# RWKV-style scan and two feed-forward blocks on one core: own terms and the one-token level of a tile from one product instead of two

## The chip, the cores and the metric

One NeuronCore of a Trainium2 chip runs the whole program. The metric is the device time of one execution in microseconds. Three runs of the kernel before gave 417.12, 417.32 and 419.42 us, so the time before is 417.32 us (median). All arithmetic is fp32 or a split of fp32 into two parts for TensorE.

## The reference

Inputs are r, k, v, w of shape (2 batches, 8 heads, 768 tokens, 48 features) and u of (8, 48).

```python
for t in range(S):
    cur = np.einsum('bhd,bhe->bhde', u[None] * kt, vt)
    y[:, :, t] = np.einsum('bhd,bhde->bhe', rt, state + cur)
    state = wt[:, :, :, None] * state + np.einsum('bhd,bhe->bhde', kt, vt)
```

So y at token t is a sum over earlier tokens s of (r_t, decayed k_s) v_s, where the decay is the product of w over the tokens strictly between s and t, and an **own term** (r_t, u k_t) v_t. For s = t - 1 no decay stands between them. After this come a normalised feed-forward block on 384 features (width 1536, relu, added to its input), and a second block with a product over the 768 tokens; neither is touched by the change.

## The kernel before

The 2 x 768 tokens are cut into 12 tiles of 128 tokens (NT = 12). In a tile the scores between tokens are built in levels c = 1, 2, 4, ... 64 (LEVELS): level c pairs the left half of every run of 2c tokens (keys) with its right half (queries). Between two levels DVE multiplies the right halves of r by the decay of a run (r_right, lines 824, 826, 821) and POOL the left halves of k (k_left, lines 559, 561, 556), in place, so the next level starts only when both are done, and both start only when TensorE (PE) has read the level before.

On PE a level (near_level, line 1120) is 16 matmuls: 4 pairs of heads, two blocks of 64 tokens, two halves of the array. Each loads 64 columns of k and streams the 32 odd columns of r in the block. The product lands in PSUM (tiles low_bank, odd_bank, high_bank), and DVE copies the entries that belong to the level into the tile near with a masked copy (select, line 868). The last level is far_level (line 1134), which ScalarE (ACT) copies to the tile score (place_blocks, line 668).

The own term has a pass of its own: ACT makes uk = u times k (own_k, line 623, four activations of 128 elements), PE multiplies uk by r in 16 matmuls of 64 columns (own_term, line 1082), and DVE copies the diagonal out with a mask over all 64 columns (own_select, line 838, 512 elements a partition). ACT then copies near to score (place_near, line 654), widens the state (widen, line 678), and PE forms y of the tile from wide and score (attend, lines 1164 and 1168) and turns k (turn_k, line 1147). A state update (gain, line 1177) and a transposition of the normalised x (turn, line 1195) follow in later slots.

The order is written out by hand for each engine: all walk through 52 slots k = 4s + j (slots_of_scan). In slot (s, j) PE does low level j of tile s, then one high level of tile s - 1; at j = 3 also the own term of tile s + 1, the attend and turn_k of tile s - 1. ACT makes uk for tile s + 1 at j = 1 and place_blocks, place_near and widen at j = 2. From slot 20 on (s = 5) each slot also holds one step of the first feed-forward block (first_product and second_product, lines 1201 to 1203) on PE; this stretch is called **beside** below, and slots 0 to 19 (tiles 0 to 4, ALONE = 4) **alone**. Weights are split in two parts by ACT (weight_hi, line 644) and POOL (weight_lo, line 571) in between. Every engine runs its own list in order.

Of the kernel before, what the change touches and what calls it, by code (L numbers as in the profile page):

```python
# [29 lines left out]
P = 128  # L30
# [3 lines left out]
Q = 64  # L34
# [9 lines left out]
def rwkv_moe_kernel(nc, rT, kT, wT, v, u, g_ln, w1, w2, w_in, w_sp, b_sp, w_out, masks, ident, out):  # L44
# [18 lines left out]
    with ExitStack() as ctx:  # L63
# [42 lines left out]
        uk = place("uk", [P, NPR, P])  # L106
# [42 lines left out]
        def low_pair(i, n):  # L149

            return (odd if i <= ALONE and n % 2 else low)[:, :, 0:Q // 2]

        def own_pair(i):

            return (high if i <= ALONE + 1 else low)[:, :, Q:2 * Q]
# [80 lines left out]
        uk_ready = sem("uk_ready")  # L236

        own_done = sem("own_done")
        low_done = sem("low_done")
        high_done = sem("high_done")  # L240
        own_placed = sem("own_placed")
# [295 lines left out]
        def _(pool):  # L537
            gp = nc.gpsimd

            def k_left(i, n):  # L540
# [8 lines left out]
                if i == n == 0:  # L549
                    pool.wait_ge(uk_ready, 1)  # L550
# [61 lines left out]
        def _(act):  # L612
            sc = nc.scalar

            def own_k(i):

                k_loaded(act, i)
                if i == 0:
                    act.wait_ge(u_loaded, 16)
                else:  # L620
                    act.wait_ge(own_done, i)
                for a in range(NPR):
                    last = sc.activation(uk[:, a, :], kin[i % 4][:, a, :], ACT.Identity, scale=ucol[:, a:a + 1])  # L623
                last.then_inc(uk_ready, 1)
# [23 lines left out]
            def place_near(i):  # L648
# [3 lines left out]
                act.wait_ge(own_placed, i + 1)  # L652
# [51 lines left out]
            own_k(0)  # L704
            for k, s, j in slots_of_scan():
# [4 lines left out]
                if j == 1 and s + 1 < NT:  # L710
                    own_k(s + 1)
# [63 lines left out]
        def _(dve):  # L775
# [29 lines left out]
            def r_right(i, n):  # L805
# [8 lines left out]
                if i == n == 0:  # L814
                    dve.wait_ge(own_done, 1)
# [13 lines left out]
            def own_select(i):  # L829

                if i == 0:
                    dve.wait_ge(near_zeroed, 2)
                    dve.wait_ge(consts_loaded, 48)
                if i >= 2:
                    dve.wait_ge(near_placed, i - 1)
                dve.wait_ge(own_done, i + 1)
                mk = msk[:, N_MASKED * Q // 2:]
                ve.copy_predicated(near[i % 2][:, :, :], mk[:, None, :].to_broadcast([P, H, Q]),
                                   own_pair(i)).then_inc(own_placed, 1)

            def select(i, n):

                c = LEVELS[n]
                if n == 0:
                    dve.wait_ge(own_placed, i + 1)
# [7 lines left out]
                if n == N_LOW - 1 and ALONE < i < NT - 1:  # L853
                    dve.wait_ge(own_done, i + 2)
# [4 lines left out]
                if c == 1:  # L859
                    dst = dst[:, :, :, 0]  # L860
                    mb = mk[:, None, :].to_broadcast([P, H, m])
                elif m == 1:
# [103 lines left out]
            for k, s, j in slots_of_scan():  # L966
# [4 lines left out]
                if k == 0:  # L971
                    own_select(0)
                if s < NT:
                    select(s, j)
                if j == 3 and s + 1 < NT:
                    own_select(s + 1)
# [94 lines left out]
        def _(te):  # L1071
            def own_term(i):

                k_loaded(te, i)
                r_loaded(te, i)
                te.wait_ge(uk_ready, i + 1)
                if 2 <= i <= ALONE + 1:
                    te.wait_ge(blocks_placed, i - 1)
                for a in range(NPR):
                    for s0 in range(0, P, Q):  # L1080
                        for e, (lo, hi) in enumerate(HALF):
                            mm = te.matmul(own_pair(i)[s0:s0 + Q, NPR * e + a, :], uk[lo:hi, a, s0:s0 + Q],
                                           rin[i % 4][lo:hi, a, s0:s0 + Q], start=True, stop=True)
                mm.then_inc(own_done, 1)

            def near_level(i, n):

                c = LEVELS[n]
                if n:
                    r_ready(te, i, n - 1)  # L1090
                    k_ready(te, i, n - 1)
                else:
                    k_loaded(te, i)
                    r_loaded(te, i)
# [3 lines left out]
                elif n < N_LOW:  # L1098
                    te.wait_ge(low_placed, N_LOW * i + n)
                    if n == 0 and i > ALONE + 1:  # L1100
# [286 lines left out]
```

## Time and profile before

| what | us |
|---|---|
| median of three runs | 417.32 |
| the profiled execution | 417.79 |
| its span, first to last instruction | 416.0 |
| PE busy | 391.5 |
| DVE, ACT, POOL busy | 226.8, 147.4, 127.4 |

The profiled execution took 417.79 us by the clock of the device, 1.8 us more than the span of its instructions. PE is the engine with the highest share, but the share is not even: the first 70 us hold most of its gaps. PE and PEld are the matmuls and the weight loads of the same engine, which overlap. Every matmul on fp32 data is counted twice (two passes), so a group of 16 shows as x32.

### The profile page before, as it was taken

The numbers are of one execution on the slowest core, as the hardware profiler recorded it, in microseconds if no ns is written. First come the engines' busy times: TensorE is split into PE (matmuls) and PEld (weight loads), VectorE is DVE, ScalarE is ACT, GpSimd is POOL, SyncE is SP. The second block draws the span as 40 slices with busy tenths as digits, with TensorE's granted clock in tenths as the row PEclk, the third lists the DMA queues.
The fourth block names the chain that finished last, engine by engine and source line by source line (L and its number), as shares of the span: only waits on it lengthen the run. The fifth ranks groups of instructions, "written<-read, shape, count | busy, mean of one in ns | idle before, by whom it ended". The sixth has DMA issues, their size and how long they took to land.

```text
span 416.0 us, 12346 instructions
## 1 busy us (share of the span) xinstructions
PE 391.5 (94%) x5244; PEld 371.0 (89%) x5244; DVE 226.8 (55%) x503; ACT 147.4 (35%) x328; POOL 127.4 (31%) x149
## 2 busy tenths in 40 slices
PE   3677788999999999999999999999999999999997
PEld 2666677999999999999999998998999899999996
DVE  2868778757576766666743334134126876624240
ACT  3334454362533333333234342222225743222121
POOL 4657667736362323232312241001003530000000
PEclk9997875999999999999999999999999999999999
DMA  6924532504201111020000210000033200010102
GB/s 199 325 63 136 172 83 96 173 2 136 73 28 45 30 47 27 4 96 4 2 2 2 70 48 0 0 2 0 2 104 125 76 2 0 2 57 3 57 19 96
DMA packets 26695, 24.99 MB, mean 60 GB/s; under 512 B 1680, under 2 KB 23440, under 8 KB 26640
## 3 DMA queue, kind: packets, MB, share of 16 engines
q1 hardware_dynamic: 26640, 24.19, 18.9%
q8 instruction: 42, 0.69, 0.7%
q14 instruction: 13, 0.11, 0.1%
HBM read 21.83 MB, written 2.36 MB: 58 GB/s over the span
## 4 chain that ended last, share of the span: by engine, by line
PE 91%; issue 3%; DVE 2%; POOL 2%; DMA 1%; ACT 0%; SPq 0%; DVEq 0%; POOLq 0%; ACTq 0%
PE odd_bank L1201 11%; PE odd_bank L1203 9%; PE odd_bank L1202 9%; PE low_bank L1120 7%; PE low_bank L1203 6%; PE low_bank L1201 6%; PE low_bank L1202 6%; PE high_bank L1201 4%; PE high_bank L1202 4%; PE high_bank L1203 4%; PE bank L1168 3%; PE bank L1203 3%; PE bank L1201 3%; PE bank L1202 3%; PE bank L1164 3%
## 5 line engine op out<-in xcount | busy, mean ns | idle before, releaser
L561 POOL TENSOR_TENSOR kin<-kin,wtot 128x256 f32<-128x256 f32 x60 | 48.5, 814 | 66.9 <-PE low_bank L1120 62.4
L1120 PEld LDWEIGHTS low_bank<-rin,kin 64*64 64x64 f32 x1728 | 31.8, 143 | 19.7 <-issue 8.1
L1120 PE MATMUL low_bank<-rin,kin 64*64 64x32 f32 x1728 | 36.3, 228 | 13.3 <-DVE rin L826 5.7
L826 DVE TENSOR_TENSOR rin<-rin,wtot 128x256 f32<-128x256 f32 x60 | 36.5, 612 | 15.5 <-PE low_bank L1120 13.4
L940 DVE SCALAR_TENSOR_TENSOR h10l<-odd_bank,h10h 128x384 fp32r<-128x384 f32 x24 | 13.4, 558 | 41.7 <-ACT h10h L700 41.7
L578 POOL TENSOR_TENSOR vrstd<-vmv,half 128x1 f32<-128x1 f32 x12 | 7.7, 644 | 72.0 <-DVE vmv L1023 72.0
L559 POOL TENSOR_TENSOR kin<-kin,win 128x256 f32<-128x256 f32 x12 | 13.1, 1089 | 49.5 <-PE low_bank L1120 45.9
L868 DVE COPY_PREDICATED near<-msk,low_bank 128x256 f32<-128x256 int32 x54 | 27.0, 552 | 0.0
L700 ACT ACTIVATE h11h<-odd_bank 128x384 fp32r<-128x384 f32 x16 | 7.9, 492 | 47.7 <-PE odd_bank L1203 47.7
L1201 PE MATMUL odd_bank<-xnT0h,ffw 128*128 128x384 f32 x66 | 24.4, 369 | 0.0
L1202 PE MATMUL odd_bank<-xnT0l,ffw 128*128 128x384 f32 x66 | 22.1, 336 | 0.0
L1203 PE MATMUL odd_bank<-xnT0h,ffw 128*128 128x384 f32 x66 | 22.1, 335 | 0.0
L1168 PE MATMUL bank<-vin,score 128*64 128x48 f32 x384 | 21.1, 245 | 0.0
L700 ACT ACTIVATE h10h<-odd_bank 128x384 fp32r<-128x384 f32 x24 | 11.8, 491 | 25.5 <-PE odd_bank L1203 25.3
L1201 PE MATMUL odd_bank<-xnT1h,ffw 128*128 128x384 f32 x54 | 19.7, 366 | 0.0
L1168 PEld LDWEIGHTS bank<-vin,score 128*64 128x64 f32 x384 | 19.5, 165 | 0.2
L1202 PE MATMUL odd_bank<-xnT1l,ffw 128*128 128x384 f32 x54 | 18.1, 336 | 0.0
L1203 PE MATMUL odd_bank<-xnT1h,ffw 128*128 128x384 f32 x54 | 18.1, 336 | 0.0
L623 ACT ACTIVATE uk<-kin,ucol 128x128 f32<-128x128 f32 x48 | 15.3, 392 | 5.7 <-DMA kin<-in_kT 2.9
L571 POOL TENSOR_TENSOR ffw<-early_stage,ffw 128x384 fp32r<-128x384 f32 x16 | 16.9, 1058 | 0.0
L1164 PE MATMUL bank<-wide,rin 128*64 128x96 f32 x160 | 16.8, 293 | 0.0
L1201 PE MATMUL high_bank<-ffw,h10h 128*128 128x384 f32 x48 | 16.1, 336 | 0.1
(244 smaller groups left out, 1138.3 us busy)
## 6 DMA issues: line engine op xcount, KB each, us to landing
kin<-in_kT SPq DMA_DIRECT2D x12, 256.0 KB, 3.3
rin<-in_rT SPq DMA_DIRECT2D x12, 256.0 KB, 4.7
win<-in_wT SPq DMA_DIRECT2D x12, 256.0 KB, 5.1
early_stage<-in_w SPq DMA_DIRECT2D x8, 384.0 KB, 5.1
vin<-in_v SPq DMA_DIRECT2D x12, 192.0 KB, 3.7
out<-ob SPq DMA_DIRECT2D x12, 192.0 KB, 1.9
stage<-in_w SPq DMA_DIRECT2D x4, 384.0 KB, 5.4
stage<-in_w_in SPq DMA_DIRECT2D x4, 384.0 KB, 3.4
```

Of the source, the lines that this page charges most:

```text
L561: last = gp.tensor_tensor(k, k, wr[:, :, :, None].to_broadcast([P, NPR, m, c]), ALU.mult)
L571: op = gp.tensor_tensor(lo[:, cs], slots[slot_of[n]][:, cs], hi[:, cs].bitcast(F32), ALU.subtract)
L623: last = sc.activation(uk[:, a, :], kin[i % 4][:, a, :], ACT.Identity, scale=ucol[:, a:a + 1])
L700: sc.activation(h1[n % 2][0][:, :], f1_bank(n)[:, 0:GT], ACT.Relu).then_inc(h1_hi_ready, 1)
L826: last = ve.tensor_tensor(r, r, wl[:, :, :, None].to_broadcast([P, NPR, m, c]), ALU.mult)
L868: ve.copy_predicated(dst, mb, src).then_inc(low_placed if n < N_LOW else middle_placed, 1)
L1120: mm = te.matmul(dst[s0:s0 + Q, NPR * e + a, :], kin[i % 4][lo:hi, a, s0:s0 + Q], r[:, :, 1, :], start=True, stop=True)
L1164: te.matmul(b_y[lo:hi, at:at + 2 * HD], rin[i % 4][:, a, lo:hi], wide[:, a, :], start=True, stop=False)
L1168: mm = te.matmul(b_y[lo:hi, at + e * HD:at + (e + 1) * HD], score[:, NPR * e + a, lo:hi], vin[i % 3][:, 2 * a + e, :], start=first(i), sto ...
L1201: te.matmul(o, wh, xh, start=first, stop=False)
L1202: te.matmul(o, wh, xl, start=False, stop=False)
L1203: return te.matmul(o, wl, xh, start=False, stop=last)
```

## The change

The own term and level c = 1 become one product. ACT writes two new tiles: k_first, which is k at even tokens and u times k at odd ones, and r_first, which is u times r at even tokens and r at odd ones. PE multiplies them in 16 matmuls of 64 columns into low_bank (first_level). At odd t the product with s = t is (r_t, u k_t) and with s = t - 1 it is (r_t, k_s); at even t the one with s = t is (u r_t, k_t). DVE takes those entries with one masked copy of 512 elements, and the mask of line 1342 gets the entries s + 1 = t at odd t. own_term, own_select and the semaphores own_done, own_placed and uk_ready go.

```diff
-            def own_k(i):
+            def first_terms(i):
                 k_loaded(act, i)
                 if i == 0:
                     act.wait_ge(u_loaded, 16)
                 else:
-                    act.wait_ge(own_done, i)
+                    act.wait_ge(low_done, N_LOW * (i - 1) + 1)
+                src, dst = halves(kin[i % 4][:, :, :], 1), halves(k_first[:, :, :], 1)
+                sc.copy(dst[0][:, :, :, 0], src[0][:, :, :, 0])
                 for a in range(NPR):
-                    last = sc.activation(uk[:, a, :], kin[i % 4][:, a, :], ACT.Identity, scale=ucol[:, a:a + 1])
-                last.then_inc(uk_ready, 1)
+                    sc.activation(dst[1][:, a, :, 0], src[1][:, a, :, 0], ACT.Identity, scale=ucol[:, a:a + 1])
+                r_loaded(act, i)
+                src, dst = halves(rin[i % 4][:, :, :], 1), halves(r_first[:, :, :], 1)
+                sc.copy(dst[1][:, :, :, 0], src[1][:, :, :, 0])
+                for a in range(NPR):
+                    last = sc.activation(dst[0][:, a, :, 0], src[0][:, a, :, 0], ACT.Identity, scale=ucol[:, a:a + 1])
+                last.then_inc(first_ready, 1)
...
-            def own_term(i):
-                k_loaded(te, i)
-                r_loaded(te, i)
-                te.wait_ge(uk_ready, i + 1)
-                if 2 <= i <= ALONE + 1:
-                    te.wait_ge(blocks_placed, i - 1)
+            def first_level(i):
+                te.wait_ge(first_ready, i + 1)
+                if i:
+                    te.wait_ge(low_placed, N_LOW * i - (1 if i <= ALONE else 0))
...
-                            mm = te.matmul(own_pair(i)[s0:s0 + Q, NPR * e + a, :], uk[lo:hi, a, s0:s0 + Q],
-                                           rin[i % 4][lo:hi, a, s0:s0 + Q], start=True, stop=True)
-                mm.then_inc(own_done, 1)
+                            mm = te.matmul(low_pair(i, 0)[s0:s0 + Q, NPR * e + a, :], k_first[lo:hi, a, s0:s0 + Q],
+                                           r_first[lo:hi, a, s0:s0 + Q], start=True, stop=True)
+                mm.then_inc(low_done, 1)
...
-                if s < NT:
+                if s < NT and j == 0:
+                    first_level(s)
+                elif s < NT:
                     near_level(s, j)
-                    if k == 0:
-                        own_term(0)
-                    if j == 3 and s + 1 < NT:
-                        own_term(s + 1)
```

On DVE, own_select (line 838) and its two calls go, and select of level 0 takes the 512 elements with the wider mask. The waits on own_done, own_placed and uk_ready in k_left, r_right, select, place_near, near_level and second_product go with them.

PE at the program's start, tile 0 and the beginning of tile 1, before (kin_53 and rin_49 are k and r of tile 0, kin_54 and rin_50 of tile 1):

```order
1 L1120 MATMUL low_bank<-rin_49,kin_53 64x32 x16
2 L1082 MATMUL high_bank<-rin_49,uk 64x64 x16
3 L1120 MATMUL odd_bank<-rin_49,kin_53 64x32 x16
4 L1120 MATMUL low_bank<-rin_49,kin_53 64x32 x16
5 L1120 MATMUL odd_bank<-rin_49,kin_53 64x32 x16
6 L1082 MATMUL high_bank<-rin_50,uk 64x64 x16
7 L1120 MATMUL low_bank<-rin_50,kin_54 64x32 x16
8 L1120 MATMUL high_bank<-rin_49,kin_53 64x32 x16
```

and in the changed kernel:

```order
1 L1067 MATMUL low_bank<-r_first,k_first 64x64 x16
2 L1097 MATMUL odd_bank<-rin_49,kin_53 64x32 x16
3 L1097 MATMUL low_bank<-rin_49,kin_53 64x32 x16
4 L1097 MATMUL odd_bank<-rin_49,kin_53 64x32 x16
5 L1067 MATMUL low_bank<-r_first,k_first 64x64 x16
6 L1097 MATMUL high_bank<-rin_49,kin_53 64x32 x16
```

Rows 1 and 2 became one group, and so did rows 6 and 7; nothing else moved.

ACT at the program's start, before:

```order
2 L703 ACTIVATE first_use<-half 128x1
3 L623 ACTIVATE uk<-kin_53,ucol 128x128 x4
4 L623 ACTIVATE uk<-kin_54,ucol 128x128 x4
5 L644 CAST ffw<-stage 128x384 x3
6 L623 ACTIVATE uk<-kin_55,ucol 128x128 x4
```

and in the changed kernel:

```order
2 L704 ACTIVATE first_use<-half 128x1
3 L618 COPY k_first<-kin_53 128x256
4 L620 ACTIVATE k_first<-kin_53,ucol 128x64 x4
5 L623 COPY r_first<-rin_49 128x256
6 L625 ACTIVATE r_first<-rin_49,ucol 128x64 x4
7 L618 COPY k_first<-kin_54 128x256
```

Four activations of a tile became ten instructions, at the same place of ACT's list.

## Rows read from the trace of the kernel before

**Rows 1.** The page: busy time, and PE, granted clock in 40 slices of the span
```profile
PE 391.5 (94%) x5244; PEld 371.0 (89%) x5244; DVE 226.8 (55%) x503; ACT 147.4 (35%) x328; POOL 127.4 (31%) x149
...
PE   3677788999999999999999999999999999999997
...
PEclk9997875999999999999999999999999999999999
```
**Rows 2.** PE by stretches: us, PE busy (instructions), granted clock, DMA share, GB/s
```profile
43.10:49.95 6.85, 5.18 (x209) 1.00 0.59 176
...
63.60:73.85 10.25, 8.94 (x179) 0.50 0.17 56
73.85:230.00 156.15, 156.15 (x2764) 1.00 0.15 45
```
**Rows 3.** Timeline of PE, beside, slot 3: start, us, what
```profile
85.56 0.67 PE L1120 MATMUL low_bank<-rin,kin 64*64 64x32 f32 x32
86.05 0.67 PE L1082 MATMUL low_bank<-rin,uk 64*64 64x64 f32 x32
86.65 0.39 PE L1164 MATMUL bank<-wide,rin 128*64 128x96 f32 x4
```
**Rows 4.** Timeline of the program's start
```profile
5.16 1.28 ACT L623 ACTIVATE uk<-kin,ucol 128x128 f32<-128x128 f32 x4 [2.84 <-DMA ucol<-in_u]
6.58 1.13 PE L1082 MATMUL high_bank<-rin,uk 64*64 64x64 f32 x32 [0.46 <-ACT uk L623]
6.62 0.99 POOL L559 TENSOR_TENSOR kin<-kin,win 128x256 f32<-128x256 f32 x1 [3.61 <-DMA win<-in_wT]
7.88 0.43 DVE L824 TENSOR_TENSOR rin<-rin,win 128x256 f32<-128x256 f32 x1 [0.98 <-PE high_bank L1082]
8.36 1.08 PE L1120 MATMUL odd_bank<-rin,kin 64*64 64x32 f32 x32 [0.64 <-DVE rin L824]
9.64 0.76 POOL L561 TENSOR_TENSOR kin<-kin,wtot 128x256 f32<-128x256 f32 x1 [2.04 <-PE odd_bank L1120]
10.87 1.08 PE L1120 MATMUL low_bank<-rin,kin 64*64 64x32 f32 x32 [1.43 <-DVE rin L826]
```
**Rows 5.** Timeline of PE: the two stops and the attend of tile 0
```profile
16.69 0.32 PE L1120 MATMUL low_bank<-rin,kin 64*64 64x32 f32 x2 [0.75 <-issue]
...
24.06 0.33 PE L1120 MATMUL low_bank<-rin,kin 64*64 64x32 f32 x3 [1.86 <-issue]
...
25.91 1.25 ACT L654 COPY score<-near 64x512 f32<-64x512 f32 x2
...
27.61 1.95 PE L1168 MATMUL bank<-vin,score 128*64 128x48 f32 x32
```
**Rows 6.** Timeline before the attends of tiles 1 and 2
```profile
39.75 0.71 ACT L678 COPY wide<-state 64x192 f32<-64x192 f32 x2
...
40.64 0.59 PE L1164 MATMUL bank<-wide,rin 128*64 128x96 f32 x4
...
52.08 0.71 ACT L678 COPY wide<-state 64x192 f32<-64x192 f32 x2
...
53.91 0.59 PE L1164 MATMUL bank<-wide,rin 128*64 128x96 f32 x4
```
**Rows 7.** The chain that ended last, 66 to 69 us
```profile
66.21 0.90 PE high_bank L1082 x31
67.11 0.69 issue
```
**Rows 8.** ACT by line and form: busy us, mean ns of one
```profile
L678 ACT COPY wide<-state 64x192 f32<-64x192 f32 x20 | 7.0, 350 | 0.4
...
L703 ACT ACTIVATE first_use<-half 128x1 f32<-128x1 f32 x1 | 0.3, 294 | 0.0
```
**Rows 9.** Timeline of ACT, the idle after the uk of tiles 5 and 7
```profile
63.70 0.58 ACT L668 COPY score<-high_bank 64x512 f32<-64x512 f32 x1 [2.27 <-PE high_bank L1134]
...
100.09 0.49 ACT L700 ACTIVATE h11h<-odd_bank 128x384 fp32r<-128x384 f32 x1 [2.94 <-PE odd_bank L1203]
```

More of the change, by code:

```diff
@@ L105, in rwkv_moe_kernel @@
         wend = [place(f"wend{q}", [P, 2 * NPR, 1]) for q in range(2)]
-        uk = place("uk", [P, NPR, P])
+        k_first = place("k_first", [P, NPR, P])
+        r_first = place("r_first", [P, NPR, P])
         near = [place(f"near{q}", [P, H, Q]) for q in range(2)]
@@ L149, in low_pair @@
         def low_pair(i, n):
+            if n == 0:
+                return low[:, :, Q:2 * Q]
             return (odd if i <= ALONE and n % 2 else low)[:, :, 0:Q // 2]
-        def own_pair(i):
-            return (high if i <= ALONE + 1 else low)[:, :, Q:2 * Q]
         def upper_bank(i, n):
@@ L703, in _ @@
             sc.activation(first_use[:, :], half[:, :], ACT.Identity, scale=half[:, 0:1])
-            own_k(0)
+            first_terms(0)
             for k, s, j in slots_of_scan():
@@ L710, in _ @@
                 if j == 1 and s + 1 < NT:
-                    own_k(s + 1)
+                    first_terms(s + 1)
                 if j == 2 and s >= 1:
@@ L844, in select @@
                 if n == 0:
-                    dve.wait_ge(own_placed, i + 1)
+                    if i == 0:
+                        dve.wait_ge(near_zeroed, 2)
+                        dve.wait_ge(consts_loaded, 48)
+                    if i >= 2:
+                        dve.wait_ge(near_placed, i - 1)
                 elif n <= N_LOW:
@@ L852, in select @@
                     level_done(dve, i - 1, N_LOW + n)
-                if n == N_LOW - 1 and ALONE < i < NT - 1:
-                    dve.wait_ge(own_done, i + 2)
+                if n == 0:
+                    mk = msk[:, N_MASKED * Q // 2:]
+                    ve.copy_predicated(near[i % 2][:, :, :], mk[:, None, :].to_broadcast([P, H, Q]),
+                                       low_pair(i, 0)).then_inc(low_placed, 1)
+                    return
                 src = low_pair(i, n) if n < N_LOW else upper_bank(i, n)
@@ L1099, in near_level @@
                     te.wait_ge(low_placed, N_LOW * i + n)
-                    if n == 0 and i > ALONE + 1:
-                        te.wait_ge(own_placed, i + 1)
-                    elif 1 <= n <= N_MIDDLE:
+                    if n <= N_MIDDLE:
                         te.wait_ge(middle_placed, N_MIDDLE * (i - 1) + n)
-                    elif n > N_MIDDLE:
+                    else:
                         te.wait_ge(blocks_placed, i)
@@ L1108, in near_level @@
                 elif n == N_LOW:
-                    if i < ALONE:
-                        te.wait_ge(own_placed, i + 2)
-                    else:
+                    if i:
                         te.wait_ge(blocks_placed, i)
```

40 lines of the change are left out of this document (6 added, 34 removed).

## The prediction

> **What bounds the kernel now.** I read the page first. PE is busy 94% of the span, but its slices are full only from the eighth on [rows 1], so there are two regimes. The next view is PE by stretches: from 73.85 to 230 us it is busy 156.15 of 156.15 us at a granted clock of 1.00, that is 2.4 GHz [rows 2]. There a PE instruction less is time less. Before that, in the alone stretch, PE, POOL, DVE and ACT pass each tile round, and only a wait on the chain counts. For this part I read the timeline and the chain of waits.
>
> The profiled execution took 417.79 us, 0.47 over the median; I sum against it and take 0.4 off at the end.
>
> **The change, part by part.**
>
> *Own groups beside.* The last group of level c = 8 starts at 85.56, the own group at 86.05, attend at 86.65 [rows 3]. A group followed by one of its own kind costs 0.49 us; the step to attend's other tile shape costs about 0.11 more and stays. Six such groups lie here, those of tiles 6 to 11, one every 20 us to 188 us. Nothing else ends late there, so 6 x 0.49 = **-2.9 us**.
>
> *The first level for level c = 1.* It has the shape of the own group, 64 x 64, and both groups last 0.67 [rows 3]: streaming 64 columns instead of 32 costs nothing a row can show. Seven tiles beside, taken at 0.0 each; from the rounding of two starts I allow 0.03 each way, +-0.2 in all.
>
> *DVE.* Twelve copies of 512 elements go, and the level 0 copy takes their shape. DVE is 55% busy [rows 1] and waits for PE where it matters, so I cost this at nothing except at the start (below), where two copies in a row stood between DVE and its next product. Were PE faster than DVE beside, the cover would be gone, but the saving there is also DVE's.
>
> *ACT.* Before, four activations took 1.28 us [rows 4]. Now there are two copies of 256 elements and eight activations of 64. A copy of 192 elements takes 0.35 and one of 512 0.62 (half of 1.25) [rows 8, 5], so 256 take 0.40. An activation with scale takes 0.39 at 128 elements (line 623) and 0.294 at one element [rows 8], and four in a row are 0.30 apart, (1.28 - 0.39) / 3; at 64 elements I take 0.25 apart. The sum is 2 x 0.40 + 8 x 0.25 = 2.8 us, +1.5 a tile. Ends: 2.2 us (pitch 0.20, copies 0.3) and 3.4 us (pitch 0.30, copies 0.5). The nearest rows speak for 2.8.
> The Trainium skill, in "ScalarE: Activation LUTs", section "Rules for kernel authors", budgets about 0.3 us per activation plus 0.83 ns an element; by it ten instructions over 1024 elements are an estimate of 3.85 us, which would make it +2.6 a tile, and it speaks against cutting work up like this. The four activations of before would come to 1.6 by it, where the trace has 1.28, so I stay with the rows.
> Outside the start ACT has room for +1.5: it stood idle 2.27 us before it placed the last level at 63.70, and 2.94 before the relu at 100.09 [rows 9]. The weight casts queued behind it move by 1.5, and POOL takes them two slots later. The new wait for r is covered too, since r of a tile is loaded more than a slot earlier. The wait on low_done holds ACT until PE has done the first level of tile i - 1, one slot back.
>
> *The start, +1.5 to +2, then repaid.* Before, level c = 1 ran from 5.04 while ACT made uk; POOL's first product began at 6.62 and only DVE waited for the own group, to 7.88 [rows 4]. Now ACT ends at 5.16 + 2.8 = 7.96, PE starts at 8.1, POOL and DVE at 8.1 + 1.30 = 9.4 (6.58 to 7.88 is 1.30), POOL takes 0.99, and the next level starts at 10.45 against 8.36: +2.1. The one after it starts 1.28 (8.36 to 9.64) + 0.76 + 0.1 later, at 12.55 against 10.87: +1.7, since DVE has one copy less before it. The last low level of tile 0 is then +1.7 too. Behind it the own group of tile 1 is gone (-0.9 at the low clock), which leaves +0.7 to +0.8 for POOL's chain.
>
> *The two stops.* In the middle of a group of 16, PE stands still with nothing waited for, 0.75 us until 16.69 and 1.86 until 24.06 [rows 5], and again 0.69 at 67.11 inside the own group of tile 5 [rows 7]. Between the first two lie 252 matmul and load records. A stop that lies at a count of instructions moves when 64 records go from every tile: at the same counts (440 and 692 records from the start) the changed list is one group later in tile 1 after the start, and inside attend of tile 0, where PE arrives some 2 us later than it had. I take it that the 1.86 goes from the chain. Then the far level of tile 0 can start when POOL's product allows, at about 22.7 instead of 24.2. The copies to score ended at 27.16 (25.91 + 1.25 [rows 5]), 3.0 after that level started; they then end at about 25.7, and attend of tile 0 starts there and not at 27.61 [rows 5]. That is -1.85, the start's +0.7 in it, with the stop gone, and between 0 and +0.7 with it unchanged. I take **-1.6**.
>
> *Tiles 1 to 3.* Attend of tile 1 starts at 40.64, and the wide copy that it needs ends at 40.46 [rows 6]; what is late next is that copy, so the own group of tile 3 gives only **-0.15**. In the next tile the copy ends at 52.79 against a start at 53.91 [rows 6], so there the group's 0.9 is on the chain, and again at 66.21 [rows 7]. But these groups run while the granted clock is 0.50, that is 1.2 GHz. It was back at 1.00 shortly before the tile's end, and if it rises at the same moment as before, other work takes the slow place and half is given back: 0.45 to 0.9 each. I take 0.7, together **-1.4**.
> The Trainium skill, in "TensorE: Matmul & The Clock Gate", section "What's actually happening", says that the moment of the rise does not follow the kernel's own start and varies from run to run; by that the 0.45 would be as likely as the 0.9. The first two of three runs here differ by 2 us, but no row says why.
>
> Sum: -2.9 - 1.6 - 0.15 - 1.4 = -6.05; 417.8 - 6.05 = 411.7, less 0.4 to the median: **411.3 us**.
>
> **The rivals.**
> *Stops stay on the chain* (the list is shifted and PE stops elsewhere, 0.7 to 1.9 us, as it did three times): 413 to 415. For: three stops in 70 us, all while weights and tiles load. Against: no stop shows later at equal counts.
> *The low clock ends earlier.* From 63.60 to 73.85 PE was busy 8.94 us at 0.50 [rows 2], longer than the other low stretches of about 6.8, and the stop at 67.11 lies in it. Without it 3.4 us could go to the high clock and 1.7 be gained, with the stop's 0.69: 408.5 to 409.5.
> *The start is not repaid.* ACT takes 3.4 or more, the chain of tiles 0 and 1 keeps +1.7 and the alone stretch gives nothing back: -2.9 + 1.7 = -1.2, 416.1, no change. Against: own groups of 0.9 stand on the chain four times.
> *The clock stays low, slower.* With one group less a tile PE is less busy before the clock rises. If it stays at 0.50 through the alone stretch, the PE work now done at 1.00, 5.18 us from 43.10 to 49.95 [rows 2] and about as much in two like stretches, takes twice the time; some 0.6 of 15 us is on the chain, +9, less 6 saved: 420. It decides once two of the three stretches are lost. Against: PE is 87% busy in the stretch before the last rise (8.94 of 10.25 [rows 2]), and the group that goes is under a seventh of a stretch.
> *The product is dearer than its rows*, as operands come from new tiles: at the widest 0.1 a group, +1.2, 412.5.
>
> **How the numbers follow.** Forecast 0.50 (409.8 to 412.8); stops stay 0.19; low clock ends earlier 0.10; dearer product 0.06; start not repaid 0.11; clock stays low 0.04. A measurement of this kernel can tell 0.5%, 2.1 us, from no change, so faster means under 415.2: the first four cases, 0.85. No change: 0.11. Slower: 0.04. The range runs from the early clock to the stops, 408.3 to 414.3; it leaves out the last two cases and an edge, under 0.2.
>
> **What would show it.** Right: PE records fall by 384 (12 x 32); attend beside starts 0.49 after the level group before it; L1067 groups last 0.67 with 0.49 between; first_terms takes 2.8 us; the second level of tile 0 starts at 10.4; attend of tile 0 starts near 25.7; PE full from about 70 us on and the later stretch 2.9 us shorter. Wrong: PE idle beside before first_level with ACT as releaser, a stop of over 1 us that the chain passes, granted clock 0.50 in over 26 us, or an ACT idle of nothing before it places the last level.

## The result and the profile after

The changed kernel took 414.35 us (median of 9 runs, 413.05 to 416.93); the kernel before, run between them, 417.65 (9 runs). The ratio of the two is **0.9947, 95% interval 0.9922 to 0.9971**. A second set gave 413.57 against 416.92, ratio 0.9944 (0.9916 to 0.9972). The gain is some 2.3 us by the ratios and 3.3 by the medians. Medians here are of all runs, ratios of those not in the slower state, which matters for one experiment (the large filling, where two of 12 are left out). The forecast was 411.3, range 408.3 to 414.3: the direction is right, the size is not, and the first set's median lies 0.05 us above the range. The profiled execution took 414.03 us, span 412.2, against 417.79 and 416.0. This pair is 3.8 us apart, 1.5 more than the ratios say; the account below adds up the pair, and those 1.5 us are differences between runs that it does not explain.

The page of the changed kernel, with the lines of [rows 1] and that of the instruction blocks:

```profile
PE 382.3 (93%) x4860; PEld 362.1 (88%) x4860; DVE 221.7 (54%) x491; ACT 164.6 (40%) x400; POOL 127.1 (31%) x149
...
PE   1676886999999999999999999999999999999997
...
PEclk9998868999999999999999999999999999999999
...
q8 instruction: 39, 0.64, 0.6%
```

PE lost 384 matmul records and 9.2 us of busy time, and 3.8 us of span came of it. The rest was idle time made elsewhere. Where, a cut of the span at the attend of each tile tells. PE by stretches, the kernel before (us, PE busy and instructions, granted clock, DMA share, GB/s); the cuts are the starts of the attends of tiles 0 to 4:

```profile
0.00:27.61 27.61, 14.63 (x433) 1.00 0.74 220
27.61:40.64 13.03, 10.02 (x299) 0.83 0.35 109
40.64:53.91 13.27, 10.73 (x316) 0.76 0.45 138
53.91:68.13 14.22, 11.21 (x315) 0.74 0.42 127
68.13:86.65 18.52, 18.52 (x358) 0.85 0.34 99
86.65:416.00 329.35, 326.34 (x3545) 1.00 0.12 36
```

And the changed kernel, cut at the same events:

```profile
0.00:27.85 27.85, 11.76 (x337) 1.00 0.73 218
27.85:41.22 13.37, 9.62 (x263) 0.88 0.37 107
41.22:54.14 12.92, 10.21 (x279) 0.76 0.46 140
54.14:67.14 13.00, 10.51 (x283) 0.76 0.47 140
67.14:85.38 18.24, 16.31 (x325) 0.96 0.32 99
85.38:412.20 326.82, 323.87 (x3385) 1.00 0.12 37
```

| stretch | measured, us | forecast, us |
|---|---|---|
| start to attend of tile 0 | +0.24 | -1.6 |
| to attend of tile 1 | +0.34 | -0.15 |
| to attend of tile 3 (two rows) | -1.57 | -1.4 |
| to attend of tile 4, and the rest | -2.81 | -2.9 |
| sum | -3.80 | -6.05 |

The whole miss stands in the first two rows. In the first stretch PE is busy 2.9 us less, and the stretch is no shorter.

The 1.00 of the first rows is not a measurement of the start: the first clock record of the trace, 1.00, comes at 29.47 us in the kernel before and at 31.15 in the changed one. Ahead of it there is none, the views print 1.00, and groups of 16 last 1.08, as they do where 0.50 is recorded (65.12 us in the kernel before), not 0.67.

**Beside.** PE's timeline, in the slots that answer to [rows 3] and in the first slot of the last tile:

```profile
84.78 0.67 PE L1097 MATMUL low_bank<-rin,kin 64*64 64x32 f32 x32
85.38 0.39 PE L1141 MATMUL bank<-wide,rin 128*64 128x96 f32 x4
...
190.32 0.69 PE L1067 MATMUL low_bank<-r_first,k_first 64*64 64x64 f32 x32
190.84 0.62 PE L1097 MATMUL low_bank<-rin,kin 64*64 64x32 f32 x32
```

From the last low level to attend there are now 0.60 us, where there were 1.09: the group cost 0.49. The first level lasts 0.69 and is followed after 0.52.

**The start.** Timeline of the changed kernel, answering to [rows 4]:

```profile
5.26 0.41 ACT L618 COPY k_first<-kin 128x256 f32<-128x256 f32 x1 [2.93 <-DMA ucol<-in_u]
...
6.87 1.08 ACT L625 ACTIVATE r_first<-rin,ucol 128x64 f32<-128x64 f32 x4
...
8.00 1.13 PE L1067 MATMUL low_bank<-r_first,k_first 64*64 64x64 f32 x32 [8.00 <-ACT r_first L625]
...
10.55 1.08 PE L1097 MATMUL odd_bank<-rin,kin 64*64 64x32 f32 x32 [1.43 <-POOL kin L554]
...
11.83 0.98 POOL L556 TENSOR_TENSOR kin<-kin,wtot 128x256 f32<-128x256 f32 x1 [1.42 <-PE odd_bank L1097]
...
12.91 1.08 PE L1097 MATMUL low_bank<-rin,kin 64*64 64x32 f32 x32 [1.28 <-DVE rin L825]
```

ACT's ten instructions took 2.69 us, from 5.26 to 7.95 (forecast 2.8). The copies last 0.41, and four activations 1.07. By the Trainium skill's budget in "ScalarE: Activation LUTs", section "Rules for kernel authors", they would have taken an estimated 3.85 us; the trace, with 2.69, lies under it and does not agree. The second level of tile 0 starts at 10.55 (forecast 10.45). The third came 0.36 later than forecast, at 12.91: POOL's product took 0.98 here and 0.76 before. It now starts within 0.04 us of DVE's product on r, where DVE's came 0.77 later before; ACT's terms are not the reason, as without them (no_own, below) it takes 0.98 too.

**The stop.** Timeline of PE behind it, up to the attend of tile 0, to be held against [rows 5]:

```profile
19.51 1.06 PE L1097 MATMUL odd_bank<-rin,kin 64*64 64x32 f32 x28 [0.92 <-DVE rin L823]
...
22.33 0.32 PE L1097 MATMUL odd_bank<-rin,kin 64*64 64x32 f32 x3 [1.76 <-issue]
...
27.85 1.42 PE L1145 MATMUL bank<-vin,score 128*64 128x48 f32 x22 [0.40 <-issue]
```

There is one stop and not two, but it is nearly as long as the longer of the two before (1.76 against 1.86), and it stands on the chain in the same tile. Counting all of PE's records from the start, those of semaphores too, PE stops before record 449 in both kernels, and in the kernel before again before 705, which is 256 further. The third stop of [rows 7] lies before record 2753, 9 x 256 after 449. An instruction block holds 16 KB by the page of the profile (0.64 MB in 39). The Trainium skill, in "Runtime: NRT & Kernel Launch", section "Instruction fetch mechanics", speaks of blocks of 16 KiB, 256 instructions, whose crossing is mostly hidden. The distance agrees; most crossings are hidden here too, but not these. The DMA queues of the changed kernel from 18 to 23 us (packets, MB, share of the 16 engines):

```profile
q1 hardware_dynamic: 1680, 1.58, 98.7%
q8 instruction: 1, 0.02, 1.4%
```

One instruction block passes in that window, among loads that fill the rest of the engines' time. The trace has the time of each such packet of q8: 42 in the kernel before and 39 in the changed one, in order one for record 449, one for 705 and so on. Held against PE's records:

| kernel, record | block landed | PE goes on | after landing | stop |
|---|---|---|---|---|
| before, 449 | 15.43 | 16.68 | 1.26 | 0.75 |
| before, 705 | 22.68 | 24.05 | 1.37 | 1.86 |
| before, 2753 | 66.43 | 67.79 | 1.36 | 0.69 |
| changed, 449 | 21.01 | 22.33 | 1.33 | 1.76 |

In the 18 traces of this case there are 694 such crossings. At none does PE go on less than 1.21 us after the landing, and all 21 stops of more than 0.25 us end 1.21 to 1.63 us after it. So a stop is PE waiting for its next block, and its length is how much later than PE's arrival that moment comes; late_loads, below, moved one.

**Tile 5.** POOL, DVE and PE of the changed kernel ahead of its first product beside:

```profile
68.45 1.21 POOL L566 TENSOR_TENSOR ffw<-early_stage,ffw 128x384 fp32r<-128x384 f32 x1
68.71 1.23 DVE L825 TENSOR_TENSOR rin<-rin,wtot 128x256 f32<-128x256 f32 x1
...
70.19 0.85 DVE L911 SCALAR_TENSOR_TENSOR xnT0l<-bank,gcol,xnT0h 128x128 fp32r<-128x128 f32 x3
...
71.19 0.63 PE L1124 MATMUL bank<-idt,kin 128*128 128x128 f32 x4 [1.55 <-DVE xnT0l L911]
71.75 0.69 PE L1067 MATMUL low_bank<-r_first,k_first 64*64 64x64 f32 x32
```

PE finished attend of tile 3 earlier and then stood 1.55 us, since DVE had still to make xnT0l. Its own product ahead of that took 1.23 us, beside a weight product of 1.21 on POOL (a like one took 0.42 to 0.43 in the start); that the one slows the other was not tried alone. So of what the shorter list gave here, VectorE took 1.55 back; the forecast had named no wait there. The lines of POOL and DVE in tile 1 read alike: DVE's product on r from 18.38 to 19.46 took 1.08, beside POOL's of 0.84.

### The profile page after: what moved, and what is told of

It is laid out like the page before. It is cut to its first block, busy times and chain, and to the rows that moved or that the text cites. A ratio compares the mean times of both kernels' runs of the same rounds, so it can differ in the third digit from the quotient of the medians.

```text
span 412.2 us, 11603 instructions
## 1 busy us (share of the span) xinstructions
PE 382.3 (93%) x4860; PEld 362.1 (88%) x4860; DVE 221.7 (54%) x491; ACT 164.6 (40%) x400; POOL 127.1 (31%) x149
## 3 DMA queue, kind: packets, MB, share of 16 engines
HBM read 21.83 MB, written 2.36 MB: 59 GB/s over the span
## 4 chain that ended last, share of the span: by engine, by line
PE 87%; DVE 4%; issue 3%; POOL 2%; ACT 1%; DMA 1%; SPq 0%; DVEq 0%; POOLq 0%; ACTq 0%
PE odd_bank L1178 10%; PE odd_bank L1180 9%; PE odd_bank L1179 9%; PE low_bank L1178 6%; PE low_bank L1180 6%; PE low_bank L1179 6%; PE low_bank L1097 5%; PE high_bank L1178 4%; PE high_bank L1180 4%; PE high_bank L1179 4%; PE bank L1178 3%; PE bank L1180 3%; PE bank L1179 3%; PE bank L1145 3%; PE bank L1141 2%
## 5 line engine op out<-in xcount | busy, mean ns | idle before, releaser
L825 DVE TENSOR_TENSOR rin<-rin,wtot 128x256 f32<-128x256 f32 x60 | 38.3, 642 | 15.7 <-PE low_bank L1097 11.7
L1097 PEld LDWEIGHTS low_bank<-rin,kin 64*64 64x64 f32 x1344 | 23.7, 138 | 9.8 <-DVE rin L825 5.2
L1097 PE MATMUL low_bank<-rin,kin 64*64 64x32 f32 x1344 | 27.1, 224 | 5.6 <-DVE rin L825 4.8
L554 POOL TENSOR_TENSOR kin<-kin,win 128x256 f32<-128x256 f32 x12 | 12.7, 1056 | 47.3 <-PE low_bank L1067 47.3
L859 DVE COPY_PREDICATED near<-msk,low_bank 128x256 f32<-128x256 int32 x42 | 19.2, 492 | 0.0
L1067 PE MATMUL low_bank<-r_first,k_first 64*64 64x64 f32 x384 | 9.4, 242 | 8.0 <-ACT r_first L625 8.0
L1067 PEld LDWEIGHTS low_bank<-r_first,k_first 64*64 64x64 f32 x384 | 7.7, 152 | 10.1 <-ACT r_first L625 8.0
```

The costliest lines, as they stand in the source:

```text
L825: last = ve.tensor_tensor(r, r, wl[:, :, :, None].to_broadcast([P, NPR, m, c]), ALU.mult)
L859: ve.copy_predicated(dst, mb, src).then_inc(low_placed if n < N_LOW else middle_placed, 1)
L1067: mm = te.matmul(low_pair(i, 0)[s0:s0 + Q, NPR * e + a, :], k_first[lo:hi, a, s0:s0 + Q], r_first[lo:hi, a, s0:s0 + Q], start=True, stop=True)
L1097: mm = te.matmul(dst[s0:s0 + Q, NPR * e + a, :], kin[i % 4][lo:hi, a, s0:s0 + Q], r[:, :, 1, :], start=True, stop=True)
```

## The experiments

Every time is the median of its runs, with the ratio to the kernel before in the same set (medians of that kernel: 416.92, 416.87, 417.01 and 416.97 in the four sets).

**The changed kernel again, and the loads moved.**

> The changed kernel once more, beside its experiments. Every theory: 414 to 415 us, a stop of 1.5 to 2 us in the middle of level c = 2 of tile 1 near 22 us, and the attend of tile 0 near 27.8. If the granted clock rises at another moment than 31.15 us, its times in the alone stretch move by up to 1 us, which shows how much of the loss is the clock's.

413.57 us (412.05 to 416.33), ratio 0.9944 (0.9916 to 0.9972). In its profile the stop before record 449 is 0.50 and not 1.76, attend of tile 0 starts at 27.20, and the span is nevertheless 414.1: the size of the stop varies between runs of one kernel. The block landed at 19.43 here and at 21.01 in the first profile.

```diff
 for i in range(1, 4):
+    if i == 3:
+        sp.wait_ge(low_done, N_LOW)
     load_w(i)
```

> The changed kernel with one wait on SyncE: the loads of tile 3 and all that SyncE issues behind them wait until level c = 8 of tile 0 is done (about 16 us). Theory A (PE stops because its next block of instructions comes by DMA behind 5 MB of data loads): the block arrives before PE needs it, the stop of 1.76 us before 22.33 is gone or under 0.3, attend of tile 0 starts at 26.3 to 26.8 instead of 27.85, and the time falls by 0.7 to 1.5. Rival B (the stop belongs to the place in the list and not to the loads): it stays at 1.5 to 2 us and the time is as before the wait. Rival C (the later loads are needed): PE or POOL waits for k, w or v of tile 3, slower by 1 or more.

> The kernel before with the same wait on SyncE as late_loads. Theory A: both its stops (0.75 us before 16.69 and 1.86 before 24.06) shrink under 0.3 and the time falls by 1 to 2 us; then the change, with the stops out of both kernels, is worth after minus before between these two. Rival B: the stops stay where they are, no change.

With the later loads the changed kernel took 415.47 (413.27 to 417.61), 0.9969 (0.9942 to 0.9996). The stop is gone and attend of tile 0 starts at 27.02 (theory A: 26.3 to 26.8), but no time came of it. In the kernel before both stops stayed, until 17.45 and 24.82 (1.42 and 1.86), and the time was 417.39, 1.0015 (0.9992 to 1.0038). The blocks explain the pair. In the changed kernel the wait brought the landing of the block of record 449 forward, from 21.01 to 18.15, ahead of PE's arrival at 20.34. In the kernel before it did not: the two blocks landed at 16.13 and 23.61, later than the 15.43 and 22.68 without it. Theory A holds on the block, and its guess that this wait would speed the block in both lists does not.

**The start shared between ACT and DVE.** DVE makes r_first of tile 0 while ACT makes k_first:

```diff
+            ve.tensor_copy(dst[1][:, :, :, 0], src[1][:, :, :, 0])
+            for a in range(NPR):
+                last = ve.tensor_scalar(dst[0][:, a, :, 0], src[0][:, a, :, 0], ucol[:, a:a + 1], None, ALU.mult)
+            last.then_inc(r_first_by_vector, 1)
```

> The changed kernel, where VectorE makes r_first of tile 0 while ScalarE makes k_first, so that five instructions stand ahead of PE and not ten. Theory A (the start lost 2.0 us to ScalarE's ten instructions): first level at 6.7 instead of 8.0, level c = 2 of tile 0 at 9.3 instead of 10.55, but the stop near 22 us swallows part, since its block comes when the loads let it: time down by 0 to 1.3. Rival (the start is hidden by later waits): first level at 6.7 all the same and no time gained at all.

413.06 us (412.3 to 414.42), 0.9923 (0.9903 to 0.9944). Its timeline:

```profile
5.26 0.74 DVE L966 TENSOR_SCALAR r_first<-rin,ucol 128x64 f32<-128x64 f32 x4
...
6.50 1.13 PE L1081 MATMUL low_bank<-r_first,k_first 64*64 64x64 f32 x32 [6.50 <-ACT k_first L621]
```

The first level starts 1.5 us earlier than in the changed kernel, attend of tile 0 at 25.92 and not 27.85, and the median is 0.5 to 1.3 lower. The intervals overlap, so that alone does not show a gain; on top of the next edit it gives 1.3 to 2.1 us (ratio 0.9915 to 0.9883 and 0.9864, below), so a part of the start's delay is on the chain to the end. A stop of 1.32 stands before record 449 here too.

**Own terms left out.** No first_terms, the first level reads k and the odd columns of r as before, and the select is the old one. This output lacks the own terms.

> The changed kernel with the own terms left out altogether: level c = 1 is the plain product of k and r again, ScalarE makes neither k_first nor r_first, and y lacks the own terms. It keeps PE's list of groups as in the change and takes ScalarE's part away. Theory A (start costs 2 us through ScalarE, the rest of its work is covered): level c = 2 of tile 0 starts at 7.9 to 8.3 (POOL's first product needs w, which lands at 6.6), about 2.3 earlier than in the change, and the time is 1.2 to 2.5 below the change, 412 us. Rival (ScalarE's +1.4 a tile also counts later): the tiles 1 to 4 get shorter by over 0.3 each beyond the start and the clock, and the time is 3 or more below the change.

412.99 us (410.57 to 413.68), 0.9895 (0.9865 to 0.9925); attend of tile 0 at 24.02. Everything that the own terms still cost in the changed kernel is about 2 us (ratios: 0.9947 less 0.9895 is 0.0052, or 2.2 us, with intervals of over 1 us each way), less than the start's share alone seemed to be in the profile, where the attend of tile 0 came 3.8 us earlier. 1.05 of the 3.8 went at once: inside this attend PE stops before record 705, until 25.81, and the attend of tile 1 is only 2.6 earlier (38.59 against 41.22). From there to the end the lead stays at 2.6 to 3.0, so no later tile got shorter by 0.3, and the rival does not hold.

**turned_lo ahead of r_right** in slot (4, 3) of DVE's list, against the wait in tile 5:

```diff
+                if (s, j) == (ALONE, 3):
+                    turned_lo(s - 2, "XT", (s - 2) // TG, (s - 2) % TG)
```

> The changed kernel, where in slot 3 of tile 4 VectorE makes the low part of the turned x before its product on r instead of behind it. Theory D (the own group's 0.9 in tile 4 was not gained because turn_k then waits for VectorE): turn_k comes at the end of attend, the PE wait of 0.8 to 1.5 on xnT0l goes, first level of tile 5 starts 0.8 to 1.4 earlier, time down by 0.5 to 1.4. Rival (another wait stands right behind it, of the first level on r or k of tile 4, or the clock): the wait goes and less than 0.3 is gained at the first feed-forward product.

413.16 us (412.93 to 414.06), 0.9915 (0.9892 to 0.9939). DVE and PE:

```profile
67.80 0.85 DVE L911 SCALAR_TENSOR_TENSOR xnT0l<-bank,gcol,xnT0h 128x128 fp32r<-128x128 f32 x3
69.39 1.12 PE L1126 MATMUL bank<-idt,kin 128*128 128x128 f32 x4
...
70.44 1.07 PE L1069 MATMUL low_bank<-r_first,k_first 64*64 64x64 f32 x32
```

The wait is gone, the first level of tile 5 starts at 70.44 rather than 71.75, and the time is about 1.3 us lower by the ratio. The two intervals overlap a little, but the same edit on top of the shared start (below) gives 1.7 to 2.5 us more, so the wait was on the chain.

> Both edits that should help, the start shared with VectorE (split_start) and lo_first. If both act where theories A and D say, 412.0 to 412.8, and the profile shows the first level at 6.5 and no wait of turn_k. If they overlap, as split_start alone.

Both edits: **410.99 us** (410.4 to 412.54), 0.9864 (0.9836 to 0.9892).

**More PE work for the clock.** Matmuls with unread results in slots j = 1 and 2 of tiles 1 to 4, ahead of attend; first 8 and 6 of them, then 2 and 2:

```diff
+                if 1 <= s <= ALONE and j in (1, 2):
+                    for _ in range(8 if j == 1 else 6):
+                        te.matmul(b_y[:, 0:Q], idt[:, :], idt[:, 0:Q], start=True, stop=True)
```

> The changed kernel with 8 and 6 further small matmuls, whose result nobody reads, in slots 1 and 2 of tiles 1 to 4, where PE waits 1.0 to 1.4 us anyway. Theory C (in the alone stretch the tiles are long because PE's granted clock stands at 0.50 for 20 to 24 us of it, and which work meets it is chance): the clock rises earlier and stays, groups of 16 take 0.67 and not 1.08 in most of 31 to 72 us, time down by 1 to 3 and the spread of the runs gets smaller. Rival (waits on POOL, VectorE and ScalarE bound the tiles, not PE's clock): clock higher, time unchanged within 0.5. Rival E (the further matmuls themselves stand in the way): slower by 0.5 to 3, at the groups behind them.

> The changed kernel with 2 further small matmuls in slots 1 and 2 of tiles 1 to 4 (their result is not read), where fill had 8 and 6 that took 3.67 and 2.8 us and stood in the way. Two take 0.46 or 0.92 us by the row of fill, less than the 1.0 to 1.4 us that PE waits there. Over its runs the changed kernel had PE's clock at 0.50 for some 22.5 us, the kernel before for 19, and a run with 10 us less of it was 3 us shorter. Theory C (the change made PE less busy and so more of the alone stretch runs at the low clock, at a price of 0.3 us for each us of it): the low clock falls below 19 us on average and the time falls by 1 or more. Rival (the moments of the clock are chance, not busyness): low clock as in the change, time within 0.5 or slower by the 0.3 to 0.5 that matmuls in the way cost.

The large one took 419.67 us (415.17 to 425.14), 1.0033 (1.0 to 1.0066), the small one 414.69 (410.68 to 415.65), 0.9933 (0.9905 to 0.9961). The time at 1.2 GHz, worked out from the mean granted clock of each run (one less the clock, times twice the span; it leaves out the start, which has no clock record), fell on the mean from 22.6 us in the changed kernel to 3.8 and to 12.7. The large filling stood in the way of the work: rival E held. The small one takes 10 us of the low clock away, and the means of all its runs and of the changed kernel's 20 are 414.26 and 414.58: a gain of 0.3, within their scatter. What the added matmuls themselves cost is in it and was not measured apart. So at most little is lost to the low clock here; that the waits for DVE, POOL and ACT cover it would explain that, but the chain of pad_before (below) shows it only from 15 to 23 us, in tiles 0 and 1.

**Matmuls of zeros ahead of the first level** (14 with 128x128 weights, 64 columns).

> The changed kernel with 14 small matmuls on zeros in the 6.5 us in which PE waits for r_first of tile 0 (their result is not read). The records call the first 31 us 1.00, but its groups last 1.08 us, as those at 0.50 do, so PE is slow there. Theory C: the first groups of tile 0 take 0.67 to 0.7, each level of tile 0 and 1 comes 0.4 earlier as long as the fast clock lasts, attend of tile 0 at 24 to 26 and time down by 1 to 2. Rival: the groups stay at 1.08, as a few matmuls don't raise it, or the stops at the blocks of instructions swallow it: time within 0.5.

413.62 us (412.46 to 416.18), 0.9928 (0.9898 to 0.9958). PE:

```profile
1.34 6.24 PE L1221 MATMUL bank<-near 128*128 128x64 f32 x28 [1.34 <-POOL near L577]
7.80 1.13 PE L1067 MATMUL low_bank<-r_first,k_first 64*64 64x64 f32 x32 [0.22 <-ACT r_first L625]
```

6.24 us of them did not shorten the groups behind, which still last 1.08. But the stop was gone and attend of tile 0 started at 26.69: the matmuls and their loads move record 449 to the head of a group. That led to the last four runs. The block of record 449 landed at 17.65 in this run, 3.4 us earlier than in the changed kernel's profile, and PE needed it only at 19.32; that alone accounts for it.

> Start shared with VectorE, low part of x first in tile 4, and 11 small matmuls on zeros before the first level. If warm_start's gain is its own, 1 to 2 us below split_lo (411.0), 409.5; if the clock falls again before tile 1, 411.

> split_lo with the 2 further matmuls of fill_small in slots 1 and 2. Theory C: 410 or less. Rival: 411 to 411.5.

412.13 us, 0.9874 (0.9833 to 0.9915), and 411.78, 0.9867 (0.9825 to 0.991): neither adds to the best version.

**The list shifted alone.** The same three kernels with 14 small matmuls of zeros in PE's idle time:

```diff
+            te.wait_ge(near_zeroed, 1)
+            for _ in range(14):
+                te.matmul(b_y[0:64, 0:32], near[0][0:64, 0, :], near[0][0:64, 1, 0:32], start=True, stop=True)
```

> The changed kernel with 14 small matmuls of zeros (64x64 weights, 32 columns, 56 records of PE with the loads, result unread) ahead of the first level, in PE's idle time of the start, where they cost nothing. They shift PE's list by 56, so that the stop's place, instruction 449, falls on the head of a group instead of its middle. Theory A (a stop costs time where it lands inside a group on the chain, and hides where PE waits anyway): no idle put down to issue of more than 0.3 us before attend of tile 0, which starts at 26.6 to 26.8 rather than 27.2 to 27.85; median 413.3 to 414.1, 0.5 to 1 below the changed kernel. Theory B (the stop is covered by the waits on ACT, DVE and POOL around it): attend of tile 0 at 27.2 or later and no gain, 414.3 to 414.8.

> The kernel before with the same 14 small matmuls ahead of its first level. Instructions 449 and 705 then both fall at the heads of groups. Theory A: both stops (0.75 at 16.69 and 1.86 at 24.06) are gone or shrink to waits that another engine sets, attend of tile 0 starts at 25.6 to 26.9 instead of 27.61, and the median is 415.7 to 416.9, 0.5 to 1.5 below the kernel before. That would mean that a part of the forecast gain, the stop of 1.86, was to be had without the change. Theory B (other work is late anyway): attend of tile 0 at 27.3 or later, median 416.8 to 417.4.

> The best version so far (the start's terms shared between ACT and DVE, turned_lo ahead of r_right in one slot) with the same 14 small matmuls ahead of the first level, so that instruction 449 falls on the head of a group. Theory A: attend of tile 0 at 25.0 to 25.3 instead of 25.5, median 410.4 to 411.0, at most 0.5 below best_again. Theory B: no difference from best_again, 411.0 to 411.5.

> The best version again, unchanged, as the measure of pad_best and to see whether the 410.99 of its first run holds. Both theories: 411.0 to 411.3 against 417.0 of the kernel before, ratio 0.985 to 0.987.

Measured: pad_after 414.46 (412.54 to 416.81), 0.9944 (0.9912 to 0.9975). pad_before 415.83 (415.38 to 416.46), 0.9978 (0.9962 to 0.9995). pad_best 411.63 (410.59 to 413.87), 0.9883 (0.9849 to 0.9917). best_again 411.6 (410.44 to 413.98), 0.9883 (0.9847 to 0.9918). Timeline of pad_after:

```profile
5.84 0.42 ACT L618 COPY k_first<-kin 128x256 f32<-128x256 f32 x1 [3.51 <-DMA ucol<-in_u]
...
20.09 1.08 PE L1097 MATMUL odd_bank<-rin,kin 64*64 64x32 f32 x32 [0.95 <-DVE rin L823]
22.23 1.08 PE L1097 MATMUL high_bank<-rin,kin 64*64 64x32 f32 x32 [1.06 <-DVE near L859]
...
27.45 1.84 PE L1145 MATMUL bank<-vin,score 128*64 128x48 f32 x30 [0.34 <-issue]
```

and of pad_before:

```profile
5.09 1.28 ACT L623 ACTIVATE uk<-kin,ucol 128x128 f32<-128x128 f32 x4 [2.77 <-DMA ucol<-in_u]
...
17.56 0.67 PE L1120 MATMUL odd_bank<-rin,kin 64*64 64x32 f32 x32 [0.46 <-DVE rin L824]
18.89 0.66 PE L1120 MATMUL high_bank<-rin,kin 64*64 64x32 f32 x30 [0.66 <-DVE near L868]
20.03 0.24 PE L1120 MATMUL high_bank<-rin,kin 64*64 64x32 f32 x2 [0.48 <-issue]
...
25.25 1.95 PE L1168 MATMUL bank<-vin,score 128*64 128x48 f32 x32
```

and of pad_best:

```profile
21.05 1.08 PE L1113 MATMUL odd_bank<-rin,kin 64*64 64x32 f32 x32 [3.28 <-issue]
...
27.25 1.95 PE L1161 MATMUL bank<-vin,score 128*64 128x48 f32 x32 [0.41 <-issue]
```

In pad_after the stop is gone, and a wait of 1.06 for DVE's copy, which the stop had covered, shows instead. u arrived 0.58 us later here (5.84 against 5.26); counted from its arrival, attend of tile 0 starts 21.61 us on and not 22.59, so **the stop of 1.76 had 1.0 on the chain** (warm_start, which has none either, gives the same: 26.69 is 18.89 after its first level, as 27.45 is after 8.56, and 27.85 is 19.85 after 8.00). The condition of theory A, no stop, held; its range for the attend held only after this correction, and its time did not: no gain.

In pad_before a stop of 0.48 is left and attend starts 2.36 earlier than at 27.61; 0.07 of it is the arrival of u. Two groups lasted 0.67 where they took 1.08, but that gave nothing, as the chain that ended last does not pass them (its pieces: start, us, what):

```profile
14.19 0.94 PE high_bank L1082 x32
15.15 0.74 DVE near L838
...
22.95 0.34 DVE rin L826
...
23.34 1.08 PE odd_bank L1120 x32
```

Between the second line and the last all its pieces are DVE's, its sequencer's or issue. The stop of 0.48 is not on it either, so **some 2.3 us is what the two stops had on the chain**. The time is lower by 0.9 us (ratio), so a part of the forecast gain was indeed to be had without the change. Of the 2.3 us the attend of tile 2 still has all (51.58 against 53.91) and that of tile 3 only 0.86 (67.27 against 68.13): in tile 5's own group, before record 2753, PE now stops for 2.08 where it stopped for 0.69. The same view, there:

```profile
64.14 2.08 issue
```

In pad_best a stop of 3.28 us stands at the head of the group; its block landed at 19.68, where that of pad_after had at 17.27. So theory A is wrong in its mechanism: not the place inside a group decides, but whether the block has landed. Shifting the list is no cure. Its time equals best_again's.

Best_again gives 411.6 and the first set 410.99: the best version stands at about 411.3, ratio 0.986 to 0.988, some 5 to 5.7 us under the kernel before. The upper end of its first interval, 0.9892, lies below the lower ends of the changed kernel's, 0.9916 and 0.9922; that of its second, 0.9918, lies between them.

## Why the prediction was wrong, point by point

**The step that failed** is the pair of terms for tile 0. The first is "I take it that the 1.86 goes from the chain", booked as -2.3 with nothing in its place. The count of instructions was used well: the stop did come one group later in tile 1. And the -2.3 was the right size for what the two stops had on the chain before (2.3 by pad_before). But the stop at the new place was priced at nothing, and it had 1.0. So the stops gave -1.3.

The second is "which leaves +0.7 to +0.8 for POOL's chain", the start repaid by the own group of tile 1. Without stops on the chain in either, pad_after against pad_before gives 27.45 - 25.25 = +2.20; less 0.75 for the arrival of u (5.84 - 5.09), it is **+1.45**, not +0.7. On the way, less the same 0.75, the fourth level of tile 0 starts 1.90 later (15.76 against 13.11) and the second level of tile 1 still 1.78 (20.09 against 17.56). The own group and its copy that went did bring DVE's first product on r of tile 1 0.8 nearer to that fourth level (3.98 us behind its start in pad_before, 3.17 in pad_after). But the product then took 1.08 and not 0.41, beside POOL's of 0.83 (the profile puts DVE, not POOL or PE, on the chain in both), and that took 0.67 back; that the one slows the other was not tried alone. Only the own group of tile 2, which ended last before attend in pad_before, repaid 0.45.

Of the miss of 1.84 in this row of the table 1.0 is the stop and 0.75 the start, and 0.1 is u, which came 0.10 later in the changed kernel's profile. That these add up is no further proof: the terms are differences of the same four starts.

**Tile 1**, -0.15 forecast, +0.34 measured. The limit named, the wide copy, is right: PE's timeline of the changed kernel has

```profile
41.22 0.59 PE L1141 MATMUL bank<-wide,rin 128*64 128x96 f32 x4 [0.76 <-ACT wide L679]
```

The group that went became a wait of 0.76. The chain ahead of the copy runs through DVE from 31.76 to 37.57; why the copy itself came later in this tile was not tried.

**Tiles 2 and 3**, -1.4 forecast, -1.57 measured. Right in sum, by luck: the two are -0.35 and -1.22 against -0.7 each, and the stop of 0.69 inside one group before [rows 7] is in the second and was not in my sum.

**Beside**, -2.9 forecast, -2.81 measured with tile 4; the last stretch alone is 2.53 for five groups, 0.5 each. Right. The sixth, in the stretch to attend of tile 4, gave 0.28, and that only because two larger things nearly cancel there: PE is busy 2.21 less (the group's 0.49, the rest a granted clock of 0.96 against 0.85) and idle 1.93 more.

**ACT's cost**, 2.8 forecast, 2.69 measured. Right. The third level of tile 0 came 0.36 later than the forecast 12.55 (whose own terms add up to 12.59), mostly by POOL's longer product.

**A wait that I did not see** is DVE's turned_lo in tile 5. Forecast was only that the group leaves; lo_first shows about 1.3 us there. It did not make the sum of that stretch wrong in the profile, because the clock rose earlier there (68.69 against 73.84), but it was a gain left lying.

**The rivals.** "Stops stay on the chain" (413 to 415, a chance of 0.19) is the nearest to what happened, with 1.0 of the 1.84; its "against", that no later stop shows at equal counts, overlooked that the third stop stood 9 x 256 records after the first. "The clock stays low" did not: 22.6 us at 1.2 GHz on the mean of 20 runs against 19.3 in 68 of the kernel before, under the 26 that was named. "The start is not repaid" held in tile 0 (+1.45 of 1.9 left, though ACT took 2.7 and not 3.4), not in the whole. The dearer product is excluded beside (0.52 against 0.49 a group).

**Open** remains what sets the moment at which a block lands: for record 449 it was 21.01 and 19.43 in two runs of one kernel, and 19.68 in a shifted one whose PE was there 3.3 us early. Each profile is one execution, and how long the stops are in the others is not recorded, so their share of the medians stays open: pad_after's profile has the attends of tiles 1 to 4 and the end 1.1 to 1.2 us earlier than the changed kernel's, and its ratio is the same. Runs of one kernel are 3 to 4 us apart, and the moments at which the granted clock falls differ between them (37.97 in the changed kernel's profile, 34.98 in after_again's, where the span is 1.9 longer); the small filling says that the time at low clock alone does not explain this.

## What to carry to other kernels

Work taken from an engine counts in full where that engine is the only one on the chain (0.49 us a group here), and only up to the next late engine where several pass the work round: look for that engine before booking the gain. A stop that the profile puts down to nothing may cover another wait: count its records, look for a stop at every multiple of their distance (256 here), hold it against the landing of the instruction blocks, and when the list gets shorter price the stop at its new place as well. A difference of two profiles is on the chain only where the chain that ended last passes it: two groups 0.4 us shorter each gave nothing here. When operands of the first step have to be made first, share them between idle engines.

## What the runs showed of the hardware

- PE's instructions come in blocks of 256 records, one packet of 16 KB on q8 each. PE went on no sooner than 1.21 us after a block had landed (694 crossings in 18 traces), and 21 times it stood waiting for that, 0.47 to 3.28 us: before record 449 in 13 traces, and before 705, 2497 and 2753. In the changed kernel the block of record 449 landed while loads kept the DMA engines 99% busy (18 to 23 us).
- DVE's product on r of 128x256 took 0.42 to 0.43 us in the first 17 us of the changed kernel and 1.08 to 1.23 beside one of POOL in tiles 1 and 5; read from traces, not tried alone.
- An fp32 group of 16 with 64 columns costs what one with 32 does: 0.52 against 0.49 us beside, 1.13 against 1.08 busy in the start.
- Matmuls of zeros for 6.24 us ahead of the work left the groups at 1.08 us; the first clock record, 1.00, comes at 30.11. In pad_before, with 3.19 us of small ones, it comes at 16.95, groups took 0.67 us at 17.56, and 0.50 follows at 20.37; in pad_after, with the same, it comes only at 33.32. What PE did between differs, and one profile each does not tell more.
